# Gated linear attention on one core: the score products in four quadrants of the array, and another order of the products of a chunk

## The chip, the core and the metric

The kernel runs on one core of a Trainium2 chip. The metric is the device time of one execution in microseconds (us), the median of several runs. The core has a matrix engine (PE, with its weight loads shown apart as PEld), a vector engine (DVE), a scalar engine (ACT), a general engine (POOL), and a queue (SP) that issues all transfers between HBM and the on-chip memory. PE writes into eight banks of PSUM, which DVE and ACT read.

## What is computed

Three stages over 2 batches of 768 tokens, with 8 heads of 64 features: a linear attention whose scores fade with distance, a feed-forward layer with a sigmoid gate, and a gated convolution layer. The change touches only the first. In the reference it reads, for each block of tokens:

```python
intra = np.einsum('bhic,bhjc->bhij', qb, kb) * Dmask[None]
intra = np.einsum('bhij,bhjd->bhid', intra, vb)
inter = np.einsum('bhid,bhde->bhie', qb * lam_pow[None], kv_state)
out[:, :, sl] = intra + inter
kb_dec = kb * rev_pow[None]
kv_state = lam_block[None, :, None, None] * kv_state + np.einsum('bhsd,bhse->bhde', kb_dec, vb)
```

The two later stages are plain matrix products with element-wise work between them.

## The kernel before

The attention works in 12 chunks of 128 tokens, six for each batch. For each chunk PE forms four groups of eight float32 products, each group in a function of its own:

- `scores(n)` (L703): keys times queries for each head, 64 rows of the array by 128 columns, 128 queries streamed. Heads lie in two rows of the array's partitions (`row` 0 and 1, 64 partitions each), four pairs `a` of heads side by side. Row 0 writes to one PSUM bank and row 1 to another.
- `update(n)` (L720): faded keys (`kdec`) times values, 128 rows by 64 columns, 64 elements streamed. It gives the new state. The last chunk of a batch has none.
- `inter(n)` (L740): the state times the faded queries (`qd`), 64 rows by 64 columns, 128 streamed. The first chunk of a batch has none.
- `attend(n)` (L755): values times the weighted scores (`pT`), 128 rows by 64 columns, 128 streamed. It adds to what `inter` has put in PSUM.

In the trace each float32 product is two weight loads and two matmuls, so a group of eight products reads x16.

Around PE, DVE multiplies the scores of the next chunk by the fading mask (`weigh`, L503), adds the new state (`new_state`, L517 and L520), and takes on the first steps of the feed-forward stage: `mix` (L527), `mix_low` (L533) and the low part of the weights `w_k` (`low`, L538). ACT copies the attention's output out of PSUM (`evacuate_x`, L316), fades the state (L324) and makes the high part of `w_k` (`high`, L330). POOL makes `kdec` (L273) and `qd` (L285). All engines run their instructions in the order in which they are written and wait on semaphores. PE's order is written out by hand: three chunks are started by single calls, and from chunk 2 on a loop calls `scores(n + 1)`, `update(n)`, `inter(n)` and `attend(n)`. The transfers of inputs (`load_qk`, `load_kv`) and of `w_k` run through one queue, six chunks deep.

After the last `attend`, PE begins the feed-forward stage with `hidden(0, 0)` (L687 to L689), which waits for the low part of the last quarter of `w_k`: in that quarter ACT's `high(wk, ..., 3)` comes behind `evacuate_x(10)`, and DVE's `low` comes behind it. From there on PE does 128x512 products in three passes.

Of the kernel before, what the change touches and what calls it, by code (L numbers as in the profile page):

```python
# [12 lines left out]
P = 128  # L13
B, H, S, D = 2, 8, 768, 64
# [25 lines left out]
def head_of(row, a):  # L40

    return 2 * a + (row ^ (a >= PAIRS // 2))
# [6 lines left out]
def build(nc, prm_in, qk_in, kv_in, w_k, w_v, w_r, w_val, w_out, out):  # L49
    with ExitStack() as ctx:  # L50
# [10 lines left out]
        def place(name, shape, at, dt=F32):  # L61
            return nc.alloc_sbuf_tensor_at(name, shape, dt, offset=at)
# [44 lines left out]
        qk = [place(f"qk_{i}", [P, 2, DM], in_at[i]) for i in range(IN_BUFS)]  # L107
# [17 lines left out]
        ps_s, ps_u = [[ps[:, 2 * i + j, :] for j in range(2)] for i in range(2)], [6, 7]  # L125
# [31 lines left out]
        def at(n):  # L157
            return n // NCB, n % NCB

        def updates(n):  # L160

            return n + 1 - (n + 1) // NCB
# [4 lines left out]
        def inters(n):  # L167

            return n - n // NCB
# [513 lines left out]
        def _(pe):  # L683
# [8 lines left out]
            def rows_of(row):  # L692
                return slice(row * D, (row + 1) * D)

            def scores(n):
                i = n % IN_BUFS
                pe.wait_ge(qk_here[i], 16 * (n // IN_BUFS + 1))
                if n >= 2:
                    pe.wait_ge(p_ready, 2 * (n - 1))
                for a in range(PAIRS):  # L700
                    cols = slice(a * P, (a + 1) * P)
                    for row in range(2):
                        last = nc.tensor.matmul(ps_s[n % 2][row][:, cols], qk[i][rows_of(row), 1, cols],  # L703
                                                qk[i][rows_of(row), 0, cols], start=True, stop=True)
                last.then_inc(scores_done, 1)

            def update(n):
                b, c = at(n)
                if c == NCB - 1:
                    return  # L710
                u = updates(n)
                i = n % IN_BUFS
                pe.wait_ge(kv_here[i], 16 * (n // IN_BUFS + 1))
                pe.wait_ge(kdec_ready, u)
                if u > 2:
                    pe.wait_ge(state_ready, u - 2)
                for a in range(PAIRS):
                    for row in range(2):
                        h, at_k = head_of(row, a), (row * PAIRS + a) * D
                        last = nc.tensor.matmul(ps[rows_of(row), ps_u[u % 2], a * D:(a + 1) * D],  # L720
                                                kdec[:, u % 2, at_k:at_k + D], kv[i][:, 1, h * D:(h + 1) * D],
                                                start=True, stop=True, skip_group_check=True)
                last.then_inc(update_done, 1)

            def place_of(n, row, a):
                return ps[rows_of(out_half(row, a)), out_banks(n)[a // 2], a % 2 * P:(a % 2 + 1) * P]

            def inter(n):
                b, c = at(n)
                if c == 0:  # L730
                    return
                pe.wait_ge(qd_ready, inters(n))
                pe.wait_ge(state_ready, updates(n - 1))
                if n < NCH - 1:
                    pe.wait_ge(x_ready, n)
                else:
                    pe.wait_ge(p_ready, 2 * n)
                for a in (0, 2, 1, 3):
                    for row in range(2):
                        last = nc.tensor.matmul(place_of(n, row, a), state[rows_of(row), n % 2, a * D:(a + 1) * D],  # L740
                                                qd[rows_of(row), inters(n) % 2, a * P:(a + 1) * P],
                                                start=(a % 2 == 0), stop=False, skip_group_check=True)
                last.then_inc(inter_done, 1)

            def attend(n):
                b, c = at(n)
                i = n % IN_BUFS
                pe.wait_ge(kv_here[i], 16 * (n // IN_BUFS + 1))
                pe.wait_ge(p_ready, 2 * n + 2)
                if c == 0 and n > 0:  # L750
                    pe.wait_ge(x_ready, n)
                for a in range(PAIRS):
                    for row in range(2):
                        h = head_of(row, a)
                        last = nc.tensor.matmul(place_of(n, row, a), kv[i][:, 1, h * D:(h + 1) * D],  # L755
                                                pT[:, n % 2, row, a * P:(a + 1) * P],
                                                start=(c == 0 and a % 2 == 0), stop=(a % 2 == 1), skip_group_check=True)
                last.then_inc(att_done, 1)
# [77 lines left out]
            for _ in range(WARM):  # L836
                nc.tensor.matmul(ps[:, 7, 0:P], warm[:, :], warm[:, :], start=True, stop=True)
            scores(0)
            scores(1)
            attend(0)  # L840
            update(0)
            scores(2)
            inter(1)
            attend(1)
            update(1)
            for n in range(2, NCH):
                if n + 1 < NCH:
                    scores(n + 1)
                update(n)
                inter(n)  # L850
                attend(n)
            for t in range(NT):
                for n in range(FT):
# [64 lines left out]
```

## Time and profile before

| | |
|---|---|
| median of 3 runs | 279.96 us (279.82 to 280.15) |
| the profiled execution | 280.36 us, of which the profile's span is 278.6 us |
| PE busy | 271.7 us (98%), 1740 matmuls and 1740 weight loads |
| DVE, ACT, POOL busy | 166.7, 126.9 and 35.1 us |
| attention, until `hidden(0, 0)` starts | 47.1 us of the span |
| TensorE clock granted, mean of the span | 1.00 of full speed |

The numbers of the profile count from the start of the span. Matmuls are pipelined: a row of the timeline tells when the first matmul of a group began and how long it took until the last one ended, and the next group begins before that, so the time that a group costs is read from start to start. "issue" is time in which an engine waited for nothing that the profile shows.

### The profile page before, as it was taken

The numbers are of one execution on the slowest core, as the hardware profiler recorded it, in microseconds if no ns is written. First come the engines' busy times: TensorE is split into PE (matmuls) and PEld (weight loads), VectorE is DVE, ScalarE is ACT, GpSimd is POOL, SyncE is SP. The second block draws the span as 40 slices with busy tenths as digits, with TensorE's granted clock in tenths as the row PEclk, the third lists the DMA queues.
The fourth block names the chain that finished last, engine by engine and source line by source line (L and its number), as shares of the span: only waits on it lengthen the run. The fifth ranks groups of instructions, "written<-read, shape, count | busy, mean of one in ns | idle before, by whom it ended". The sixth has DMA issues, their size and how long they took to land.

```text
span 278.6 us, 4270 instructions
## 1 busy us (share of the span) xinstructions
PE 271.7 (98%) x1740; PEld 226.0 (81%) x1740; DVE 166.7 (60%) x253; ACT 126.9 (46%) x229; POOL 35.1 (13%) x30
## 2 busy tenths in 40 slices
PE   8799998999999999999999999999999999999996
PEld 7688886888888888888888888888888888888885
DVE  5658998975976103456786635436987599415000
ACT  2337668867794114356821134558226404512121
POOL 1686660008600000000000000000000000000000
DMA  6999995000000000000000000260000000300223
GB/s 235 409 405 411 408 402 235 0 0 0 2 0 0 0 2 0 0 0 2 1 0 0 4 0 0 72 231 0 0 0 2 0 0 0 115 38 0 113 78 113
DMA packets 7506, 22.83 MB, mean 82 GB/s; under 512 B 960, under 2 KB 1216, under 8 KB 7488
## 3 DMA queue, kind: packets, MB, share of 16 engines
q1 hardware_dynamic: 7488, 22.57, 21.1%
q8 instruction: 14, 0.23, 0.3%
q14 instruction: 4, 0.03, 0.0%
HBM read 19.42 MB, written 3.15 MB: 81 GB/s over the span
## 4 chain that ended last, share of the span: by engine, by line
PE 95%; DMA 2%; issue 1%; SPq 0%; POOL 0%; ACT 0%; POOLq 0%
PE ps L687 27%; PE ps L688 27%; PE ps L689 27%; PE ps L703 4%; PE ps L755 4%; PE ps L740 2%; PE ps L720 2%; DMA kv<-in_kv 2%; POOL kdec L273 0%; SPq L204 0%; SPq L214 0%; ACT out_sb L400 0%; POOLq L282 0%; POOLq L270 0%
## 5 line engine op out<-in xcount | busy, mean ns | idle before, releaser
L687 PE MATMUL ps<-xk_h,wk_h 128*128 128x512 f32 x96 | 37.4, 390 | 0.8 <-issue 0.8
L689 PE MATMUL ps<-xk_h,wk_l 128*128 128x512 f32 x96 | 37.4, 389 | 0.0
L687 PE MATMUL ps<-kk_h,wv_h 128*128 128x512 f32 x96 | 37.3, 389 | 0.0
L688 PE MATMUL ps<-kk_l,wv_h 128*128 128x512 f32 x96 | 37.3, 389 | 0.0
L689 PE MATMUL ps<-kk_h,wv_l 128*128 128x512 f32 x96 | 37.3, 389 | 0.0
L688 PE MATMUL ps<-xk_l,wk_h 128*128 128x512 f32 x96 | 37.3, 389 | 0.0
L542 DVE SCALAR_TENSOR_TENSOR kk_f<-ps,ring 128x512 f32<-128x512 f32 x24 | 16.6, 691 | 29.0 <-ACT ring L353 29.0
L566 DVE SCALAR_TENSOR_TENSOR gate<-x,prm,gate 128x512 f32<-128x512 f32 x48 | 32.6, 747 | 0.0
L353 ACT ACTIVATE ring<-ps 128x512 f32<-128x512 f32 x24 | 14.3, 598 | 31.6 <-PE ps L689 31.5
L370 ACT ACTIVATE gate<-x,prm 128x512 f32<-128x512 f32 x12 | 8.7, 725 | 42.6 <-DVE x L552 42.6
L687 PEld LDWEIGHTS ps<-xk_h,wk_h 128*128 128x128 f32 x96 | 18.0, 188 | 4.7 <-issue 1.0
L687 PEld LDWEIGHTS ps<-kk_h,wv_h 128*128 128x128 f32 x96 | 18.0, 188 | 3.8
L688 PEld LDWEIGHTS ps<-kk_l,wv_h 128*128 128x128 f32 x96 | 18.0, 188 | 3.8
L688 PEld LDWEIGHTS ps<-xk_l,wk_h 128*128 128x128 f32 x96 | 18.0, 188 | 3.8
L689 PEld LDWEIGHTS ps<-xk_h,wk_l 128*128 128x128 f32 x96 | 18.0, 188 | 3.7
L689 PEld LDWEIGHTS ps<-kk_h,wv_l 128*128 128x128 f32 x96 | 18.0, 188 | 3.7
L552 DVE TENSOR_TENSOR x<-ps,r 128x512 f32<-128x512 f32 x12 | 8.3, 691 | 20.5 <-PE ps L689 20.5
L688 PE MATMUL ps<-w_l,gh 128*128 128x512 f32 (+1 forms) x52 | 19.4, 373 | 0.0
L689 PE MATMUL ps<-w_h,gl 128*128 128x512 f32 (+1 forms) x52 | 19.4, 373 | 0.0
L687 PE MATMUL ps<-w_h,gh 128*128 128x512 f32 (+1 forms) x52 | 19.4, 373 | 0.0
L503 DVE TENSOR_TENSOR pT<-ps,dec 128x512 f32<-128x512 f32 x24 | 15.4, 682 | 6.4 <-PE ps L703 6.3
L547 DVE TENSOR_TENSOR kk_l<-kk_f,kk_h 128x512 fp32r<-128x512 f32 x24 | 18.0, 752 | 1.8 <-ACT kk_h L357 1.8
(71 smaller groups left out, 507.5 us busy)
## 6 DMA issues: line engine op xcount, KB each, us to landing
qk<-in_qk SPq DMA_DIRECT2D x12, 512.0 KB, 10.2
kv<-in_kv SPq DMA_DIRECT2D x10, 512.0 KB, 11.0
out<-out_sb SPq DMA_DIRECT2D x11, 256.0 KB, 2.0
wk_raw<-in_w_k SPq DMA_DIRECT2D x4, 512.0 KB, 11.8
wv_raw<-in_w_v SPq DMA_DIRECT2D x4, 512.0 KB, 14.7
wr_raw<-in_w_r SPq DMA_DIRECT2D x2, 512.0 KB, 13.2
w_raw<-in_w_val SPq DMA_DIRECT2D x2, 512.0 KB, 4.4
w_raw<-in_w_out SPq DMA_DIRECT2D x2, 512.0 KB, 6.9
```

What stands on the lines that cost most here:

```text
L353: nc.scalar.activation(ring[:, n % 4, :], ps[:, bank_of("mlp", t, n), :], ACT.Relu).then_inc(relu_ready, 1)
L370: nc.scalar.activation(like(t, gate[t][:, k, :]), x_cols(t, k, HALO), ACT.Copy, scale=prm[:, col:col + 1]).then_inc(tap0, 1)
L503: nc.vector.tensor_tensor(pT[:, n % 2, row, :], ps_s[n % 2][row], dec[:, row * PAIRS:(row + 1) * PAIRS, :].rearrange("p a i -> p (a i)"), ...
L542: nc.vector.scalar_tensor_tensor(out=kk_f[:, n, :], in0=ps[:, bank_of("mlp", t, n), :], scalar=0.0, in1=ring[:, n % 4, :], op0=ALU.max, op ...
L547: nc.vector.tensor_tensor(kk[1][:, n, :], kk_f[:, n, :], f32(kk[0][:, n, :]), ALU.subtract).then_inc(kk_lo, 1)
L552: nc.vector.tensor_tensor(x_cols(t, m, 1), like(t, ps[:, bank_of("mlp", t, FT + KT + m), :]), like(t, r[:, m, :]), ALU.mult).then_inc(x2_r ...
L566: nc.vector.scalar_tensor_tensor(out=like(t, gate[t][:, k, :]), in0=x_cols(t, k, HALO - j), scalar=prm[:, col:col + 1], in1=like(t, gate[t ...
L687: nc.tensor.matmul(to, left(0), right(0), start=(i == 0), stop=False)
L688: nc.tensor.matmul(to, left(0), right(1), start=False, stop=False)
L689: done = nc.tensor.matmul(to, left(1), right(0), start=False, stop=(i == last))
L703: last = nc.tensor.matmul(ps_s[n % 2][row][:, cols], qk[i][rows_of(row), 1, cols], qk[i][rows_of(row), 0, cols], start=True, stop=True)
L755: last = nc.tensor.matmul(place_of(n, row, a), kv[i][:, 1, h * D:(h + 1) * D], pT[:, n % 2, row, a * P:(a + 1) * P], start=(c == 0 and a % ...
```

## The change

`scores(n)` now splits each product by the keys of the chunk into two halves of 64. Each half uses 64 rows by 64 columns of the array, and the two halves write to the lower and the upper 64 partitions of the same bank. There are 16 products in a group instead of 8, with the same 128 queries streamed in each; the results lie in PSUM where they lay. In the loop from chunk 2 on, `inter(n)` now comes ahead of `update(n)`. The calls for chunks 0 and 1 keep their order, and no wait is added or removed.

```diff
                 for a in range(PAIRS):
                     cols = slice(a * P, (a + 1) * P)
                     for row in range(2):
-                        last = nc.tensor.matmul(ps_s[n % 2][row][:, cols], qk[i][rows_of(row), 1, cols],
-                                                qk[i][rows_of(row), 0, cols], start=True, stop=True)
+                        for half in range(2):
+                            keys = slice(a * P + half * D, a * P + (half + 1) * D)
+                            last = nc.tensor.matmul(ps_s[n % 2][row][rows_of(half), cols], qk[i][rows_of(row), 1, keys],
+                                                    qk[i][rows_of(row), 0, cols], start=True, stop=True,
+                                                    skip_group_check=True)
                 last.then_inc(scores_done, 1)
...
                 if n + 1 < NCH:
                     scores(n + 1)
+                inter(n)
                 update(n)
-                inter(n)
                 attend(n)
```

PE's queue before, at chunk 4 and the first group of what follows. The names `qk_99` and `kv_104` are buffers; L703 is `scores(5)`, L720 `update(4)`, L740 `inter(4)`, L755 `attend(4)`; the last two rows but one are `scores(6)` and `inter(5)` (chunk 5 has no update). The sizes are those of each product's output.

```order
18 L703 MATMUL ps<-qk_99 128x128 x8
19 L720 MATMUL ps<-kv_104,kdec 64x64 x8
20 L740 MATMUL ps<-qd,state 64x128 x8
21 L755 MATMUL ps<-pT,kv_104 64x128 x8
22 L703 MATMUL ps<-qk_94 128x128 x8
23 L740 MATMUL ps<-qd,state 64x128 x8
24 L755 MATMUL ps<-pT,kv_105 64x128 x8
```

The same place on PE now (L705 is `scores`, L743 `inter`, L723 `update`, L758 `attend`):

```order
18 L705 MATMUL ps<-qk_99 64x128 x16
19 L743 MATMUL ps<-qd,state 64x128 x8
20 L723 MATMUL ps<-kv_104,kdec 64x64 x8
21 L758 MATMUL ps<-pT,kv_104 64x128 x8
22 L705 MATMUL ps<-qk_94 64x128 x16
23 L743 MATMUL ps<-qd,state 64x128 x8
24 L758 MATMUL ps<-pT,kv_105 64x128 x8
```

`scores` has twice the products, each of half the output, and `inter` has moved from behind `update` to behind `scores`. The queues of DVE, ACT, POOL and SP are the same as before.

## Rows read from the trace of the kernel before

**Rows 1.** Page, engines' shares of the chain; busy time by stretch, the later stages.

```profile
PE 95%; DMA 2%; issue 1%; SPq 0%; POOL 0%; ACT 0%; POOLq 0%
...
core 0: us, PE busy (x) PEld busy (x) DVE busy (x) ACT busy (x) POOL busy (x), PEclk, DMA share, GB/s
47.12:276.10 228.98, 228.91 (x1020) 189.84 (x1020) 129.95 (x190) 101.42 (x171) 10.22 (x4) 1.00 0.06 23
```

**Rows 2.** Chain of waits in order of time (start, us, what), end of the attention.

```profile
43.15 1.02 PE ps L755 x16
44.18 0.33 issue
...
46.34 0.78 issue
47.12 0.47 PE ps L687
```

**Rows 3.** Timeline of ACT and DVE (start, us, what) at the same place.

```profile
44.23 0.59 ACT L316 COPY x<-ps 128x512 f32<-128x512 f32 x1 [0.45 <-PE ps L755]
44.71 1.05 ACT L330 CAST wk_h<-wk_raw 128x1024 fp32r<-128x1024 f32 x1
...
45.79 1.22 DVE L538 TENSOR_TENSOR wk_l<-wk_raw,wk_h 128x1024 fp32r<-128x1024 f32 x1 [0.25 <-ACT wk_h L330]
```

**Rows 4.** Timeline of PE, chunk 4 and the scores behind it.

```profile
21.07 1.16 PE L703 MATMUL ps<-qk 64*128 64x128 f32 x16
22.16 0.69 PE L720 MATMUL ps<-kv,kdec 128*64 128x64 f32 x16
22.77 0.67 PE L740 MATMUL ps<-qd,state 64*64 64x128 f32 x16
23.37 1.09 PE L755 MATMUL ps<-pT,kv 128*64 128x128 f32 x16
24.39 1.45 PE L703 MATMUL ps<-qk 64*128 64x128 f32 x16
```

**Rows 5.** Timeline of PE, chunk 6, where update and attend are neighbours.

```profile
28.49 0.69 PE L720 MATMUL ps<-kv,kdec 128*64 128x64 f32 x16
29.00 1.05 PE L755 MATMUL ps<-pT,kv 128*64 128x128 f32 x16
29.98 1.16 PE L703 MATMUL ps<-qk 64*128 64x128 f32 x16
```

**Rows 6.** Timelines of PE and of its weight loads, groups with a pause in them.

```profile
17.12 1.77 PE L703 MATMUL ps<-qk 64*128 64x128 f32 x16
...
31.68 1.05 PE L740 MATMUL ps<-qd,state 64*64 64x128 f32 x16
...
18.19 0.52 PEld L703 LDWEIGHTS ps<-qk 64*128 64x128 f32 x6 [0.33 <-issue]
...
32.07 0.42 PEld L740 LDWEIGHTS ps<-qd,state 64*64 64x64 f32 x14 [0.20 <-issue]
...
38.95 0.13 PEld L720 LDWEIGHTS ps<-kv,kdec 128*64 128x64 f32 x1 [0.30 <-issue]
```

**Rows 7.** Queues: 15.8 to 17.0, 29.45 to 30.6, 36.35 to 37.5 (packets, MB, share).

```profile
q8 instruction: 1, 0.02, 5.7%
...
q8 instruction: 1, 0.02, 6.0%
...
q8 instruction: 1, 0.02, 5.8%
```

**Rows 8.** Busy time and instruction counts by stretch, around the pauses (columns as above).

```profile
15.80:18.18 2.38, 2.26 (x42) 1.72 (x33) 0.68 (x2) 0.93 (x3) 2.38 (x3) 1.00 1.03 391
29.45:32.06 2.61, 2.61 (x46) 2.06 (x42) 2.61 (x6) 1.36 (x5) 1.19 (x1) 1.00 1.00 397
36.35:38.94 2.59, 2.44 (x44) 2.01 (x41) 2.59 (x4) 1.77 (x6) 2.18 (x2) 1.00 1.05 407
18.19:24.90 6.71, 6.71 (x124) 5.65 (x124) 4.24 (x7) 3.76 (x11) 4.64 (x5) 1.00 1.02 410
```

**Rows 9.** The same view, from update(4) to the end of attend(10).

```profile
22.16:44.18 22.02, 21.86 (x402) 18.14 (x400) 21.91 (x30) 15.56 (x36) 12.72 (x10) 1.00 1.03 406
```

**Rows 10.** Timelines of POOL and DVE: mix beside POOL's work, and without it.

```profile
23.68 1.27 POOL L285 TENSOR_TENSOR qd<-qk,qdec 128x512 f32<-128x512 f32 x1 [0.19 <-DMA qk<-in_qk]
...
23.81 2.36 DVE L527 SCALAR_TENSOR_TENSOR xk_f<-x,om,xk_f 128x512 f32<-128x512 f32 x2
...
50.22 2.73 DVE L527 SCALAR_TENSOR_TENSOR xr_f<-x,om,xr_f 128x512 f32<-128x512 f32 x4
```

## Prediction

> **What bounds the kernel now.** I read the shares of the chain first: 95% of the span is PE. Then the later stages: from 47.12 to 276.10 us PE is busy for 228.91 of 228.98 us [rows 1]. The change leaves those products alone, so it can move the end only by moving the start of `hidden(0, 0)` at 47.12, and the rest follows one for one. That start is read from the chain of waits and the two timelines beside it [rows 2, 3]. `attend(10)` ends at 44.18; ACT then copies its output (from 44.23), makes the high part of the last quarter of `w_k` (44.71 to 45.76), DVE makes the low part (45.79 to 47.01), and PE starts at 47.12. DVE had waited 0.25 us for ACT. So a later `attend(10)` delays everything by as much; an earlier one gives at most about 0.25 us before DVE's own work is the bound, unless DVE is earlier too. And DVE is nearly full: busy for 21.91 of the 22.02 us from 22.16 to 44.18, as PE is with 21.86 [rows 9]. PE and DVE are two almost equal bounds.
>
> **What the change takes away on PE.** The products of a chunk use three shapes of the array: 64x128 for `scores`, 64x64 for `inter`, 128x64 for `update` and `attend`. In chunk 4 each group has a neighbour of another shape, and the groups cost, from start to start, 1.09 (`scores`), 0.61 (`update`), 0.60 (`inter`) and 1.02 us (`attend`), 3.32 together [rows 4]. In chunk 6 `update` and `attend` stand side by side in one shape: there `update` costs 0.51 and `attend` 0.98 [rows 5]. A change of shape less saves 0.10 + 0.04, about 0.15 us.
>
> The new `scores` has 32 matmuls of 64x64. `inter` is the row for that shape: 16 of them cost 0.60, while 16 of `attend`, with as many streamed elements in each, cost 1.02. That fits four at a time against two: four more rounds for 0.42 us, 0.11 us a round, and in each group 0.16 on top. The new `scores` then has eight rounds, as `attend` has: 0.87 us, and with a change of shape only ahead of it 0.93. `inter` behind it, without a change ahead of it, costs 0.55. A chunk becomes 0.93 + 0.55 + 0.51 + 0.98 = 2.97 us against 3.32: 0.35 saved. Chunks 2, 3, 4, 7, 8, 9 and 10 have all four groups in the new order: 7 x 0.35 = 2.5. Chunks 1 and 5 gain only between `scores` and `inter`, 0.2 each; chunk 6, without `inter`, 0.1. **Sum: 3.0 us** saved on PE until `attend(10)` ends, if nothing else changes.
>
> **What the change adds on PE.** It adds instructions: 16 weight loads and 16 matmuls for each chunk. That would be free if each were ready when the array is, but some are not. Four groups in this stretch take too long, with a pause inside: `scores(4)` takes 1.77 where a normal one shows 1.16 (0.61 lost), `scores(6)` 1.45 (0.29), `inter(7)` 1.05 against 0.67 (0.38) [rows 4, 6], and `update(9)` breaks off before its last weight load at 38.95 [rows 6], for another 0.4. No semaphore wait stands inside a group. What stands near each is a single 16 KB packet on the instruction queue: it starts after 15.80, 29.45 and 36.35 [rows 7], and PE resumes at 18.19, 32.07 and 38.95 [rows 6], each time 2.4 to 2.6 us later. Between one pause and the next (18.19 to 24.90) there are 124 weight loads and 124 matmuls [rows 8]; with semaphore instructions that is one block of 256 instructions of 64 bytes, 16 KB. I read it so: the next block is asked for only about 80 instructions ahead (33 + 42, 42 + 46 and 41 + 44 recorded from the packet to the pause [rows 8], some of them under way already), and it is usable 2.5 us after. PE eats those 80 in about 2.1 us now, so it pauses for the rest.
>
> The new chunk has 160 recorded instructions in 2.97 us instead of 128 in 3.32: 18.5 ns each, not 26. Eighty then last 1.5 us, or 1.1 to 1.3 where they lie in the dense new `scores` (64 in 0.87 us), and the pause grows to 1.0 to 1.4 us. I take 1.1. The number of pauses grows too. From the first (17.8) to the end of `attend(10)` there are now 250 + 802 recorded instructions, less the few between 22.16 and 24.90 counted twice: about 950 [rows 8, 9]. The 12 `scores` add 384, of which 128 lie ahead of the place where the first pause falls, so that it falls in or behind `scores(3)`. From there it is about 950 + 384 = 1330 instructions, so five more pauses follow the first: six in place of four. **Sum: 6 x 1.1 = 6.6 us against 1.7 now, 4.9 us more.**
>
> What bounds this cost? From below: the pauses stay at 0.43 us each, as the mean of the four is now, and only two are added (0.9). From above: 2.6 us with only 60 instructions ahead, 1.5 us each, 9.0 in all. I choose 1.1, because three resumptions lie within 0.2 us of the same delay after their packet, although the pauses themselves differ by 0.3: the delay is the constant, not the pause.
>
> The Trainium skill says otherwise: in "Runtime: NRT & Kernel Launch", section "Instruction fetch mechanics", the sequencer fetches the next 16 KiB block (256 instructions) while it runs the current one, and the crossing is mostly hidden. The block size agrees with the trace; that it is hidden does not, since PE pauses for 0.61 us in `scores(4)`. By that rule this cost would be nothing, which is the second rival below.
>
> **The rest.** The order of `inter` and `update`: `new_state(n)` on DVE now waits for an `update` that ends some 0.5 us later in its chunk. DVE has `weigh` of 1.2 us ahead of it and `update` ends 0.55 + 0.51 us after the scores, so this costs nothing as long as no pause falls between them; where one does, DVE waits about a pause less 0.2. That is already in PE's delay, since DVE then has nothing else that PE waits for. `inter(n)` waits for `new_state(n - 1)`, and `update(n)` is now queued behind that wait. POOL's `kdec` and `qd` follow the arrival of keys and queries and are there earlier. ACT and the queue of transfers see the same order.
>
> **Sum.** 4.9 - 3.0 = +1.9 us on the end of `attend(10)`. It passes through the copy, the high part and the low part unchanged. The profiled execution would go from 280.36 to 282.2, and the median, 0.4 below it, from 279.96 to about 281.8 us.
>
> **Rivals.**
>
> *The pauses stay as they are* (the block is asked for earlier when PE runs faster). Then PE is early: -3.0 + 0.9 = -2.1 us at `attend(10)`. DVE decides then. Its unbroken work begins with the scores of chunk 5, which come some 0.9 us earlier (1.1 gained until there, 0.2 lost to pauses). But DVE's `mix` takes 2.36 us for two beside POOL, and 2.73 for four without it [rows 10]: the two engines hold each other up there, and POOL's times are set by the transfers, which do not move. DVE, earlier, meets more of POOL's work. I give back half: -0.4 us, 279.5. This is the case that is not slower; it holds if a pause after a dense stretch stays under about 0.7 us (six of them then cost 4.2, 2.5 more than now). Chance 0.2.
>
> *Instructions cost nothing at all.* The pauses vanish: 3.0 + 1.7 = 4.7 us of PE's time are free, DVE starts 1.7 us earlier, and the end is bound by it: 278.4 us. The skill's rule above would lead here. The rows speak against it. Chance 0.07.
>
> *The quadrants do not overlap as in `inter`*, because all four of one head pair stream from the same two buffers, say two at a time over 16 rounds: 0.87 us more for each of some ten chunks, +8.7 and more, 288 us or above. Against it: `inter` does it in the same shape. Chance 0.04.
>
> **How the numbers follow.** The forecast with its growing pauses has 0.69; its own range, from pauses of 0.8 to 1.4 us, is 280.3 to 283.6. The range given adds the lower cases down to 279.3. A difference of 0.2% (0.56 us) is about what a measurement can tell from none. Slower by more than that: nearly all of the forecast (0.65) and the third rival (0.03). Within it: most of the first rival and a little of the forecast, 0.18. Faster: the second rival and the rest of the first, 0.14.
>
> **What would show it.** In the profile after: a `scores` without a pause costs 0.93 us from start to start, `inter` 0.55, `update` 0.51, `attend` 0.98. Six groups before the end of `attend(10)` hold a pause of around 1.1 us, the first near 14 us, each ending 2.4 to 2.6 us after an instruction packet starts. `attend(10)` ends near 46.1 and `hidden(0, 0)` starts near 49.0. If the pauses are 0.4 us, the second part is wrong and DVE's chain ends last; if a chunk without a pause costs 3.3, the first part is.

## The result, and the profile after

The changed kernel takes 285.9 us (median of 5 runs, 285.76 to 286.08) against 279.82 us for the kernel before (5 runs): a ratio of 1.0214, with a 95% interval of 1.0200 to 1.0228. The forecast was 281.8 us and the range ended at 283.6. The direction was right and the size was not: 6.1 us more instead of 1.9. (An execution more than 1.5% above the fastest of its kernel is left out of the ratios in this document, but not out of the medians and ranges.)

The later stages are unchanged, as [rows 1] was read. From the start of `hidden(0, 0)` on, PE is busy for 228.90 of 228.95 us; the columns are those of the same view before.

```profile
PE 92%; issue 3%; POOL 0%; DVE 0%; ACT 0%
...
52.69:281.64 228.95, 228.90 (x1020) 189.91 (x1020) 129.75 (x190) 101.98 (x172) 10.20 (x4) 1.00 0.06 23
```

`hidden(0, 0)` starts at 52.69 instead of 47.12, 5.57 us later, and the span is 5.5 us longer (284.1 against 278.6). That is all of the difference between the two profiled executions (285.9 and 280.36 us), and it comes from the attention; the median has 0.5 us more, because the profiled execution before was a slower one than its median. "issue", 1% of the chain before, is now 3%. First the chain of waits (start, us, what) at the end of the attention, then the timelines of ACT and DVE, which answer to [rows 2, 3]:

```profile
48.61 1.14 PE ps L758 x16
49.75 1.06 PE ps L743 x16
50.81 1.86 PE ps L758 x16
52.67 0.02 issue
...
50.29 1.05 ACT L330 CAST wk_h<-wk_raw 128x1024 fp32r<-128x1024 f32 x1
...
51.37 1.23 DVE L538 TENSOR_TENSOR wk_l<-wk_raw,wk_h 128x1024 fp32r<-128x1024 f32 x1 [1.15 <-ACT wk_h L330]
```

`attend(10)` ends at 49.75 instead of 44.18: again 5.57 us. DVE, which had waited 0.25 us for the last high part of `w_k` [rows 3], now waits 1.15 us. ACT and DVE follow as before, and DVE's last low part ends at 52.60.

One thing is new here: the granted clock of TensorE falls to 0.50, the lower of its two levels, from 49.1 to 52.4 us, after the longest of the pauses described below (2.2 us, ending at 47.56). The columns are those of [rows 1]:

```profile
49.10:52.40 3.30, 3.30 (x40) 2.56 (x36) 2.15 (x2) 1.53 (x2) 0.00 (x0) 0.50 0.00 0
```

So `attend(10)` takes 1.31 us where it took 1.09, and `inter(11)` and `attend(11)` behind it fill the time until 52.67, where PE stood idle before. This adds 0.2 us and not 6: the executions of the changed kernel whose mean granted clock was 1.00 took as long (285.85 to 286.08 us).

In chunks without a pause the array is as fast as forecast. PE's timeline, the second half of `attend(3)` and chunk 4, which answers to [rows 4]:

```profile
20.67 0.66 PE L758 MATMUL ps<-pT,kv 128*64 128x128 f32 x8 [1.15 <-issue]
21.25 1.10 PE L705 MATMUL ps<-qk 64*64 64x128 f32 x32
22.18 0.62 PE L743 MATMUL ps<-qd,state 64*64 64x128 f32 x16
22.73 0.69 PE L723 MATMUL ps<-kv,kdec 128*64 128x64 f32 x16
23.24 1.05 PE L758 MATMUL ps<-pT,kv 128*64 128x128 f32 x16
24.22 1.10 PE L705 MATMUL ps<-qk 64*64 64x128 f32 x32
```

From start to start: `scores` 0.93, `inter` 0.55, `update` 0.51, `attend` 0.98, a chunk 2.97 us. These are the numbers of the forecast. The pauses are another matter. The parts of PE's timeline that they interrupt (the row of 20.67 above is the end of the first):

```profile
18.90 0.61 PE L758 MATMUL ps<-pT,kv 128*64 128x128 f32 x8
...
25.14 0.40 PE L743 MATMUL ps<-qd,state 64*64 64x128 f32 x5
27.13 0.65 PE L743 MATMUL ps<-qd,state 64*64 64x128 f32 x11 [1.59 <-issue]
27.71 1.09 PE L758 MATMUL ps<-pT,kv 128*64 128x128 f32 x16
...
33.80 0.66 PE L743 MATMUL ps<-qd,state 64*64 64x128 f32 x14 [1.24 <-issue]
...
40.64 0.27 PE L758 MATMUL ps<-pT,kv 128*64 128x128 f32 x1 [1.73 <-issue]
...
47.56 0.44 PE L743 MATMUL ps<-qd,state 64*64 64x128 f32 x4 [2.22 <-issue]
```

There are five. `attend(3)` takes 2.35 us from start to start (18.90 to 21.25) instead of 0.98, so it loses 1.37; `inter(5)` loses 2.02 (25.14 to 27.71, less 0.55). Read the same way, `inter(7)`, `attend(8)` and `inter(10)` lose 1.7, 2.0 and 2.6. The five cost 9.7 us.

What do these pauses have in common with those of [rows 6 to 8]? The busy times and counts of PE (first bracket) and of its weight loads (second), first from just before an instruction packet to the end of the pause, then from the end of one pause to the end of the next:

```profile
18.20:20.66 2.46, 1.31 (x36) 1.01 (x28) 1.50 (x3) 0.38 (x2) 2.43 (x3) 1.00 1.02 400
24.80:27.12 2.32, 0.74 (x25) 0.49 (x18) 2.32 (x4) 1.86 (x4) 0.23 (x2) 1.00 1.03 410
31.35:33.79 2.44, 1.21 (x34) 0.96 (x35) 2.25 (x5) 2.05 (x6) 0.32 (x1) 1.00 1.03 410
38.05:40.63 2.58, 0.86 (x15) 0.62 (x12) 2.58 (x5) 0.43 (x1) 2.00 (x2) 1.00 1.03 405
45.05:47.55 2.50, 0.29 (x8) 0.05 (x2) 1.21 (x2) 1.36 (x3) 0.00 (x0) 1.00 0.39 149
20.67:27.12 6.45, 4.87 (x125) 4.11 (x125) 4.69 (x7) 5.10 (x11) 2.56 (x3) 1.00 1.02 386
27.13:33.79 6.66, 5.43 (x125) 4.50 (x125) 6.47 (x9) 3.67 (x9) 3.49 (x3) 1.00 1.03 415
33.80:40.63 6.83, 5.11 (x125) 4.35 (x125) 5.51 (x8) 2.48 (x6) 5.19 (x4) 1.00 1.03 404
40.64:47.55 6.91, 4.70 (x125) 3.92 (x125) 5.30 (x7) 4.96 (x12) 1.29 (x1) 1.00 0.79 311
```

and the instruction queue in the stretch 24.8 to 25.9 us; the stretches 18.2 to 19.3, 31.3 to 32.5, 38.0 to 39.3 and 45.0 to 46.3 have one packet of 16 KB each too:

```profile
q8 instruction: 1, 0.02, 5.5%
```

Two things stayed. A packet starts 2.3 to 2.6 us before PE resumes, and there are 250 recorded instructions between two resumptions. One did not: the instructions that PE does between the packet and its pause were 75 to 88 before [rows 8]; in the five pauses now they are 64, 43, 69, 27 and 10. And one more number stayed that I had not looked at: the time from one resumption to the next, 6.5 to 6.9 us, while before it was 6.7 to 7.2 (18.19, 24.9, 32.07, 38.95, [rows 6, 8]). Here the packet starts 4.1 to 4.4 us after the last resumption (20.67 to 24.8, 27.13 to 31.3, 33.80 to 38.0, 40.64 to 45.0), although PE has done very different shares of its block by then. So it does not start a fixed number of instructions ahead of the boundary, as the prediction had it.

This gives a new theory, called **supply** below: while the loads run, PE gets a block of 256 instructions only every 6.5 to 7.2 us, which is 26 to 29 ns for each of the 250 recorded ones, and the time follows their number. Before, a chunk's 128 recorded instructions take 3.5 us at the 6.9 us a block of that trace, a little more than its work on the array (3.32), so the limit was met but hardly seen. Now there are 160, which take 4.3 us at 6.7 us a block, against 2.97 of work.

### The profile page after: what moved, and what is told of

Read it like the earlier page. It is cut to its first block, busy times and chain, and to the rows that moved or that the text cites. A ratio compares the mean times of both kernels' runs of the same rounds, so it can differ in the third digit from the quotient of the medians.

```text
span 284.1 us, 4654 instructions
## 1 busy us (share of the span) xinstructions
PE 270.6 (95%) x1932; PEld 225.1 (79%) x1932; DVE 167.4 (59%) x253; ACT 126.4 (44%) x229; POOL 34.8 (12%) x30
## 4 chain that ended last, share of the span: by engine, by line
PE 92%; issue 3%; POOL 0%; DVE 0%; ACT 0%
PE ps L687 27%; PE ps L688 27%; PE ps L689 27%; PE ps L758 4%; PE ps L705 3%; PE ps L743 2%; PE ps L723 2%; POOL qd L285 0%; DVE qdec L596 0%; ACT out_sb L400 0%
## 6 DMA issues: line engine op xcount, KB each, us to landing
kv<-in_kv SPq DMA_DIRECT2D x10, 512.0 KB, 11.5
```

## Experiments

### Is it the order or the quadrants, and is it the number of instructions?

**The quadrants alone.** The changed kernel with the order of before:

```diff
-                inter(n)
                 update(n)
+                inter(n)
                 attend(n)
```

> The scores in quadrants, with the order of before (update ahead of inter): the same instructions as in the changed kernel, but two more changes of the array's shape in a chunk. Theory S (supply): while inputs are loaded, PE gets a block of 256 instructions only every 6.6 to 7.0 us, counted from the moment it begins the block before, so the time follows the number of instructions and not their cost on the array: 285.4 to 286.4 us, pauses shorter than in the changed kernel by what the chunk is longer. Theory of the prediction (a block is asked for some 80 instructions ahead and takes 2.5 us): the order's gain of 0.15 us in 7 chunks is lost and nothing else moves, 1 us more than the changed kernel, 286.9 us.

Measured: 285.79 us (285.43 to 286.06), ratio 1.0203, interval 1.0184 to 1.0221. It is as slow as the changed kernel, although each full chunk has two more changes of shape. PE's timeline of this kernel, where pauses end, and the start of `hidden(0, 0)`:

```profile
15.34 0.44 PE L705 MATMUL ps<-qk 64*64 64x128 f32 x4 [1.13 <-issue]
22.21 0.66 PE L758 MATMUL ps<-pT,kv 128*64 128x128 f32 x8 [1.37 <-issue]
28.34 0.65 PE L743 MATMUL ps<-qd,state 64*64 64x128 f32 x11 [0.95 <-issue]
35.37 0.62 PE L723 MATMUL ps<-kv,kdec 128*64 128x64 f32 x14 [1.54 <-issue]
42.19 0.27 PE L758 MATMUL ps<-pT,kv 128*64 128x128 f32 x1 [1.29 <-issue]
...
52.54 0.47 PE L687 MATMUL ps<-xk_h,wk_h 128*128 128x512 f32 x1 [1.32 <-issue]
```

These five pauses are mostly shorter than those of the changed kernel, since the array works longer, and they end 6.1 to 7.0 us apart. What the array takes more, the pauses take less. A sixth, of 0.38 us, ends at 47.64, only 5.45 us after the fifth; by then the loads are ending (the transfer engines are 0.72 busy from 44 to 46 us and 0.13 from 46 to 48).

**The order alone.** The kernel before with the loop of the changed one:

```diff
                     scores(n + 1)
+                inter(n)
                 update(n)
-                inter(n)
                 attend(n)
```

> The new order with the scores as before: 0.1 to 0.15 us less of the array in 7 chunks, and no instruction more. Theory S: the blocks come as before, so the pauses grow by what the array saves, 279.6 to 280.1 us. If instead the groups' cost on the array decided, 0.7 to 1.0 us less: 278.9 to 279.2 us.

Measured: 280.32 us (279.81 to 280.9), ratio 1.0006, interval 0.9992 to 1.0020. No change (0.2 us above the range of supply, and a gain was forecast by the other theory), while the array's work fell by 0.15 us in each of seven chunks. `scores(6)` shows where it went: 0.29 us lost before, now a break of its own of 0.81 us in PE's timeline.

```profile
24.37 0.71 PE L703 MATMUL ps<-qk 64*128 64x128 f32 x6
25.89 0.93 PE L703 MATMUL ps<-qk 64*128 64x128 f32 x10 [0.81 <-issue]
```

**Quadrants with the old number of instructions.** The changed kernel with the upper half of the keys left out from chunk 2 on:

```diff
-                        for half in range(2):
+                        for half in range(2 if n < 2 else 1):
```

> The changed kernel, leaving out the products of the upper 64 keys of each chunk from chunk 2 on: 8 products of 64x64 in a group of scores, as many instructions as in the kernel before. The array still needs eight rounds for a group (two quadrants work instead of four), so its own work stays 0.93 us. Theory S (supply by blocks of 256 instructions): the pauses shrink to those of the kernel with the new order alone, 279.6 to 281.0 us. If the 64x64 shape or its change of pace made the pauses, or if the array's own work decided: 285 to 286.3 us as in the changed kernel.

Measured: 281.33 us (281.29 to 281.55), ratio 1.0048, interval 1.0031 to 1.0064: 0.3 us above what was expected, but 4.6 us below the changed kernel, with the same shape and the same eight rounds a group. In the timeline a group without a pause shows that the array's work stayed (`scores(7)`, then `update(6)` behind it, 1.02 us from start to start with a change of shape at both ends):

```profile
26.17 1.09 PE L705 MATMUL ps<-qk 64*64 64x128 f32 x16
27.19 0.69 PE L723 MATMUL ps<-kv,kdec 128*64 128x64 f32 x16
```

So 320 recorded instructions fewer bring back three quarters of the loss. This is the cleanest of the comparisons: array shape, order and array time are held, the count is not. What is not held is that four quadrants work at once; here it is two. The kernel with few loads below has all four and loses nothing like 6 us.

Part of what is left is another wait. Before `inter(7)` PE stands for 1.72 us at the border of two groups; by the code it waits there for the state of chunk 6, which DVE has written at 31.40 (timelines of PE and DVE):

```profile
31.50 0.67 PE L743 MATMUL ps<-qd,state 64*64 64x128 f32 x16 [1.72 <-issue]
...
30.99 0.41 DVE L517 COPY state<-ps 128x256 f32<-128x256 f32 x1
```

This stretch also shows what supply does not explain. Two of its packets start some 9 us apart, at 26.1 and 35.1, with the transfer engines full, and the pause that ends at 37.67 follows from the late second one. What starts a packet is therefore not time alone.

**The same number of instructions without quadrants.** The kernel before, with each score product split by its queries:

```diff
-                        last = nc.tensor.matmul(ps_s[n % 2][row][:, cols], qk[i][rows_of(row), 1, cols],
-                                                qk[i][rows_of(row), 0, cols], start=True, stop=True)
+                        for half in range(2):
+                            queries = slice(a * P + half * D, a * P + (half + 1) * D)
+                            last = nc.tensor.matmul(ps_s[n % 2][row][:, queries], qk[i][rows_of(row), 1, cols],
+                                                    qk[i][rows_of(row), 0, queries], start=True, stop=True)
```

> The order and the array shape of before (64x128), but each score product split by its queries into two of 64 streamed columns: 16 products in a group and as many instructions as in the changed kernel, without quadrants. Theory S: the number of instructions decides, 285.3 to 286.5 us, with pauses of 1 to 2 us. If quadrants were the cause: within 1 us of before, plus what 32 weight loads of 128 columns cost beyond the 0.9 us of a group, at most 0.9 us a chunk without any pause.

Measured: 289.67 us (287.97 to 292.5), ratio 1.0323, interval 1.026 to 1.0387. Both expectations missed. Its trace is of the longest execution (292.5 us), so only sizes are taken from it: `scores` took nearly 2 us.

```profile
19.66 2.05 PE L705 MATMUL ps<-qk 64*128 64x64 f32 x32
21.64 0.69 PE L722 MATMUL ps<-kv,kdec 128*64 128x64 f32 x16
```

That is 1.98 us for 32 weight loads of 128 columns and their matmuls, 62 ns a pair; the array itself became the bound, at 4.2 us a chunk (19.66 to 23.88). The run doesn't tell the theories apart. It agrees with supply in so far as 160 instructions in 4.2 us, 26 ns each, is about the pace of the supply, and no group behind 17 us shows a pause inside.

### What sets the time from one resumption to the next?

**Few loads.** In both kernels, the queries, keys and values of chunks 6 to 11 are left out but for 16 columns, and `w_r` and `w_v` are loaded late:

```diff
+                width = DM if n < IN_BUFS else 16
-                sp.dma_start(qk[n % IN_BUFS][:, :, :], qk_in[n]).then_inc(qk_here[n % IN_BUFS], 16)
+                sp.dma_start(qk[n % IN_BUFS][:, :, 0:width], qk_in[n, :, :, 0:width]).then_inc(qk_here[n % IN_BUFS], 16)
...
+            sp.wait_ge(att_done, NCH - 1)
             for i in range(2):
                 load_weight(wr_raw, w_r, i, wr_here)
```

> The changed kernel, leaving out nearly all of the queries, keys and values of chunks 6 to 11 (16 of 512 columns are loaded) and with the loads of w_r and w_v issued only near the end of the attention, so that from about 23 us on the transfer engines have nearly nothing to do. Its products are all made. Theory S1 (it is the loads that hold the instruction packets back): the delay from the end of one pause to the next instruction packet falls from 4.2 to 4.4 us to under 2, the pauses after 25 us vanish or fall under 0.3 us, hidden(0, 0) starts near 46 us, 279 us in all. Theory S2 (the cycle of 6.7 us is the instruction queue's own): pauses as in the changed kernel, 285.5 to 286.3 us.

> The kernel before with the same loads left out and moved. Theory S1: its pauses after 25 us (0.4 us at 32 and 39 us) vanish; DVE is then the bound, 279.0 to 279.8 us. Theory S2: pauses as before, 279.5 to 280.0 us.

Measured: the changed kernel 279.86 us (ratio 1.0006, 0.9984 to 1.0028), the one before 279.07 us (ratio 0.9957, 0.9941 to 0.9974). The loss of 6 us is down to 0.8 us between the two; pauses that end at 15.9 and 21.86 are left in the changed one. Theory S2 is refuted. The same view and stretch for the changed kernel with few loads, and for the changed kernel as it is:

```profile
30.00:40.00 10.00, 10.00 (x256) 8.44 (x252) 10.00 (x15) 7.15 (x18) 7.43 (x6) 1.00 0.20 58
```

```profile
30.00:40.00 10.00, 7.67 (x191) 6.50 (x188) 8.48 (x14) 5.01 (x13) 6.20 (x5) 1.00 1.03 407
```

With the transfer engines 20% busy PE does 508 recorded instructions in 10 us without idling; with them full it does 379. DVE is now the one that is busy all the time. In the kernel with few loads, the last pause of this kind ends at 21.86, and the next packets lie in 23.8 to 24.9 and 28.6 to 29.7: the first 2.0 us after the pause instead of 4.1 to 4.4.

```profile
21.86 0.66 PE L762 MATMUL ps<-pT,kv 128*64 128x128 f32 x8 [1.07 <-issue]
...
q8 instruction: 1, 0.02, 5.5%
```

**Shorter pieces.** Perhaps the instruction packet waits for its turn behind pieces of the loads. Here every load is cut in two:

```diff
-                sp.dma_start(qk[n % IN_BUFS][:, :, :], qk_in[n]).then_inc(qk_here[n % IN_BUFS], 16)
+                for part in range(2):
+                    sp.dma_start(qk[n % IN_BUFS][:, part, :], qk_in[n, :, part, :]).then_inc(qk_here[n % IN_BUFS], 16)
```

> The changed kernel with every load of queries, keys, values and of w_k, w_r and w_v cut into two transfers, so that a partition's piece is 2 KB instead of 4 KB (and 1 KB for the last chunk of a batch). Same bytes, same products. Theory S1a: the instruction packet waits on its transfer engine for whole turns of the loads' queue, so its delay after a pause falls with the length of a turn, from 4.2 to 4.4 us to 2 to 3 us; the pauses fall by 1 to 2 us each and the time to 279.5 to 282 us. Theory S1b: it waits for something else that loads hold back (their share of the memory, say): 285.5 to 286.3 us.

> The kernel before with the same loads cut in two. Theory S1a: its four pauses (1.7 us) vanish, but DVE is then the bound: 279.0 to 279.8 us. Theory S1b: 279.7 to 280.1 us.

Measured: 289.59 us (ratio 1.0338, 1.0317 to 1.0359) and 282.03 us (1.0064, 1.004 to 1.0088). All four expectations missed: both are slower. The loads fell from 404 to 385 GB/s, and what that cost shows at the start, not in the pauses behind 24 us. In the trace of the changed kernel `attend(0)` starts at 9.70 us instead of 8.05, since it waits for its values, and behind that wait the granted clock is 0.50 until 13.3 us; by the end of the next pause (24.24 instead of 20.67) all of the 3.6 us is lost, and `hidden(0, 0)` starts 3.6 us later too. In the trace of the kernel before, `scores(4)` starts 2.7 us later than it did (of which 1.8 are left at `hidden(0, 0)`), again behind a wait for inputs and a stretch at the lower clock (the view of [rows 8]):

```profile
7.75:14.00 6.25, 6.25 (x62) 5.91 (x64) 2.98 (x8) 1.43 (x5) 3.75 (x4) 0.50 1.03 383
```

How much of the rest is the clock's is open. What the experiment was made for is answered by the stretch behind 24 us: the pauses did not get shorter, and the time from one resumption to the next stayed at 6.9 us:

```profile
30.70 0.65 PE L751 MATMUL ps<-qd,state 64*64 64x128 f32 x11 [1.59 <-issue]
37.64 0.66 PE L751 MATMUL ps<-qd,state 64*64 64x128 f32 x14 [1.51 <-issue]
44.49 0.27 PE L766 MATMUL ps<-pT,kv 128*64 128x128 f32 x1 [1.73 <-issue]
```

The length of the pieces is not it, as far as a factor of two can tell.

**Fewer loads under way.** SP waits, before each load, until the one so many before it has landed (three here, then two, four, six):

```diff
+            sent = []
+            def in_flight(sem_, at_least):
+                if len(sent) >= 3:
+                    sp.wait_ge(*sent[-3])
+                sent.append((sem_, at_least))
             def load_qk(n):
                 free(n)
+                in_flight(qk_here[n % IN_BUFS], 16 * (n // IN_BUFS + 1))
```

> The changed kernel, with SP waiting before each load of inputs or weights until the third before it has landed: at most three transfers of 512 KB are under way at a time, instead of up to eight. Same transfers, same order; three should still keep the engines full (one lands every 1.3 us and takes 2 to 4 us). Theory Q (the instruction packet waits behind what the loads have already queued): the delay from the end of a pause to the next instruction packet falls from 4.2 to 4.4 us to 2 to 3 us and the pauses by as much, 279.5 to 282 us. Theory R (it is the load on the engines or on the memory itself, however little is queued): delay and pauses as in the changed kernel, 285.5 to 286.5 us.

> The same with at most two transfers under way. The loads may fall below their full rate. Theory Q: the delay falls further, under 2.5 us, pauses under 0.5 us, and what is lost or gained is the loads' (279 to 282 us). Theory R: the delay falls only as far as the engines' busy share falls; 284 to 286.5 us.

> The kernel before with at most three transfers under way. Theory Q: its four pauses vanish, DVE is then the bound, 279.0 to 279.8 us. Theory R: 279.7 to 280.3 us, no change.

> The changed kernel with at most four loads under way. With three, the loads fell to 300 GB/s and PE took instructions faster than 38 per us without pauses, so the supply follows how full the transfer engines are. Theory Q (queued loads hold the instruction packet back, and four already keep the engines full): full rate, 400 GB/s, and pauses under 1 us, 280 to 283 us. Theory R (only idle time of the engines lets the packet through): as far as the loads reach the full rate the pauses come back, as far as they don't PE waits for loads; 285 to 287 us.

> The same with at most six under way. Theory Q: pauses between those of three and of eight, 281 to 284 us. Theory R: the loads run at the full rate and the pauses are those of the changed kernel, 285.5 to 286.5 us.

Measured: the changed kernel takes 297.76 us with two under way (ratio 1.0633), 287.64 with three (1.0263), 283.47 with four (ratio 1.0111, 1.0074 to 1.0148; single runs 281.3 to 289.9) and 285.76 with six (1.0203, 1.0187 to 1.0218); the kernel before takes 287.43 with three (1.0272). With two and three under way, both theories missed for both kernels. Four lies between the two ranges (by its ratio 283.1 us), and six agrees with theory R. The busy times and counts from 14 to 44 us (last two columns: busy share of the transfer engines, GB/s), first of the changed kernel with three under way:

```profile
14.00:44.00 30.00, 21.74 (x528) 18.77 (x528) 17.14 (x29) 14.10 (x36) 15.39 (x13) 0.94 0.85 292
```

With four:

```profile
14.00:44.00 30.00, 26.21 (x660) 22.02 (x655) 24.62 (x34) 18.07 (x46) 20.78 (x16) 1.00 0.97 355
```

With six:

```profile
14.00:44.00 30.00, 24.55 (x580) 20.60 (x576) 20.55 (x31) 15.51 (x41) 17.86 (x15) 0.94 1.03 407
```

And as it is, with no limit:

```profile
14.00:44.00 30.00, 24.29 (x618) 20.65 (x620) 23.43 (x34) 16.62 (x43) 19.17 (x16) 1.00 1.03 404
```

With six, the engines are as full as ever and nothing is gained. PE's smaller count there is a matter of the clock, which was 0.50 from 22.7 to 26.1 us, behind a pause that ended at 22.39. That makes a test which nobody planned: the array worked at half its pace for half of a block, and the block still took the same 6.5 us, with the pause at its end down to about 0.5 us (start and end are two resumptions):

```profile
22.39:28.90 6.51, 6.43 (x125) 5.35 (x125) 3.44 (x5) 4.04 (x10) 3.76 (x3) 0.74 1.02 408
```

With four, the engines are at 0.97, the loads at 355 GB/s, and PE does 1315 recorded instructions instead of 1238; by the ratios the changed kernel gains 2.9 us by carrying its data more slowly. With three, no group behind 14 us has a pause inside, and PE waits for queries instead (timeline of PE):

```profile
33.61 1.10 PE L715 MATMUL ps<-qk 64*64 64x128 f32 x32 [3.27 <-DMA qk<-in_qk]
```

So the loads hold the instruction packets back. Whether it is the last few per cent of the engines' time or the loads already queued that lets a packet through earlier stays open: at four both change together, and at six neither has changed.

**Could the order win, with the queue shorter?** The order alone with six loads under way:

> The scores of before in the new order, with at most six loads under way: could this beat both kernels? Theory Q: no pauses, the array's gain of 1 us reaches DVE's bound, 279.0 to 279.6 us. Theory R: 279.8 to 280.6 us, as with the order alone.

Measured: 280.00 us (ratio 0.9999, 0.9987 to 1.0011). No change. None of the versions with full inputs beat the kernel before.

## Why the prediction was wrong

- **What bounds the kernel, and that the end follows `attend(10)` one for one**: right. Both moved by 5.57 us.
- **The array's gain**: right. 2.97 us a chunk were measured as forecast; from `scores(3)` to the end of `attend(10)` it is 2.8 us.
- **The pauses as the price of more instructions**: right in kind. They are what makes the kernel slower, the packet 2.4 to 2.6 us ahead of each resumption was seen again (2.3 to 2.6), and so were the 250 recorded instructions of a block.
- **The size of a pause**: this is the step that failed, and the term of the sum that it feeds. The next block was taken to be "asked for only about 80 instructions ahead", a fixed number, which PE would use up in 1.1 to 1.5 us, and a pause of 1.1 us followed. In the three pauses I had counted, 75 to 88 instructions were the same fact as 4.3 to 4.6 us after the last resumption (24.90 to 29.45 and 32.07 to 36.35), since the pace of PE was nearly the same each time. In the changed kernel the count fell to 64, 43, 69, 27 and 10 while the delay stayed at 4.1 to 4.4 us, and the pauses became 1.4 to 2.6 us: 9.7 us for five instead of 6.6 for six. The term was 3 us too small, and the measured 9.7 lies above even its upper bound of 9.0, which still had 60 instructions between packet and pause.
- **The number of pauses**: six forecast, five seen, and this hid a part of the error: six of the measured size would have been 11.6 us. The first boundary, near 14 us, passed without one: its packet had started at 11.5, while PE waited 0.9 us for POOL's `qd`. In the kernel with the quadrants alone, where that wait is missing, this pause is there (1.13 us, ending at 15.34).
- **The sum, again**: from `scores(3)` (13.65 before, 13.96 now) to the end of `attend(10)`: 2.8 us less of the array, 1.8 us of old pauses and a wait gone, 9.7 us of new pauses and 0.2 us of the lower clock, +5.3; with the 0.3 us from the start it is the 5.6 us. The working of the forecast with five pauses of 1.9 us gives 9.7 - 1.7 - 3.0 = +5.0; six of that size would have given 6.9.
- **The reading that was missing**: the prediction used the time from a packet to the end of its pause. The time from one resumption to the next, 6.7, 7.2 and 6.9 us in [rows 6, 8], stood in the same rows. An estimate from it alone, the 288 recorded instructions that are added from `scores(3)` on at 27.7 ns each, is 8.0 us against the 5.3 measured: the right direction, and too much, since nothing holds PE back in the first chunks of that stretch and behind the last resumption. Between the starts of `scores(4)` and `scores(10)` it fits better: 896 instructions now at 26.9 ns are 24.1 us (23.92 measured), 704 before at 27.7 ns are 19.5 (19.90 measured).
- **The rivals**: "the pauses stay as they are" and "instructions cost nothing" are refuted while the loads run. With few loads the second is nearly true after 25 us. There DVE is busy for all of 30 to 40 us, as that rival has it, but the kernel takes 279.86 us and not 278.4. "The quadrants do not overlap" is refuted by the 0.93 us.
- **The Trainium skill**, "Runtime: NRT & Kernel Launch", section "Instruction fetch mechanics", says that the next block is fetched while the current one runs and that the crossing is mostly hidden. The first half fits all the runs: the packet for the next block starts during the current one. The second fits the stretches in which the transfer engines are mostly idle (0.20 busy in the kernel with few loads), and not those in which they are full.

## What to carry to other kernels

When the matrix engine's products are short, count its instructions as well as its columns: here a block of 256 instructions came only every 6.1 to 7.2 us while the loads filled the transfer engines, some 27 ns for each recorded instruction, and the new `scores` asks for 64 of them in 0.93 us, where that pace allows 1.7. Look for rows that break off inside a group with no wait, and measure from one such break to the next: if that time stays when the work between changes, it is a supply rate. Splitting products to fill the array better adds instructions, so its place is where the data has already arrived; but no run here shows it to pay, since even with few loads the changed kernel took 279.86 us against 279.07.

## What the hardware showed that I had not expected

The loads hold instruction packets back: the delay from a pause's end to the next packet was 4.1 to 4.4 us in the changed kernel at a busy share of 1.02 to 1.03 and 2.0 us at about 0.5. Cutting the loads to half-length pieces did not change it, nor did limiting them to six under way. The packet itself hardly suffers: 5.5% of sixteen engines for 1.1 us are 0.97 us for its 16 KB, and in an empty stretch (48.9 to 49.9 us, 5.5%) it took 0.88. It starts late. What makes it start stays open. In the later stages, with the engines all but idle, packets start at 61.1 and 89.9 us, 28.8 us apart, which is the time that PE takes there for its 250 recorded instructions, and no pause appears; and in the kernel with the lower keys alone two were some 9 us apart at full load.

The quadrants are as good as they look: 32 matmuls of 64x64 in 0.93 us. And a 64x128 product with only 64 streamed columns gains nothing: its group of 32 weight loads of 128 columns took 1.98 us, more than the 1.09 us of the 16 loads with 128 streamed columns. A pause or a wait can also be followed by a lower clock: the granted clock was 0.50 from 49.1 us behind the pause of 2.2 us in the changed kernel, and from 22.7 us behind one of 1.9 us with six loads under way. Other pauses as long were not followed by it.
